# The choice of experts and the third routed tile, in another order

## The reference

```python
logits = x @ w_gate                       # 8 per token
local_gate = sigmoid(x @ w_local)
for s in range(S):
    fresh_e = argmax(logits[b, s])
    e = fresh_e if s == 0 or local_gate[b, s] < 0.5 else prev_e
    prev_e = e
    p = softmax(logits[b, s])
    out[b, s] = p[e] * (relu(x[b, s] @ w1[e]) @ w2[e])
```

## Time and profile before

| | us |
|---|---|
| median of 3 runs | 627.2 (627.11 to 627.49) |
| the profiled execution | 627.01 |
| its span, first to last instruction | 625.0 |
| PE busy | 608.4 (97%) |
| DVE busy | 410.3 (66%) |
| ACT busy | 321.1 (51%) |
| POOL busy | 176.5 (28%) |

### The profile page before, as it was taken

One profiled execution on the slowest core, in us unless ns is written; L12 is line 12 of the kernel. 1 busy time (PEld: TensorE's weight loads), 2 busy tenths in 40 slices (PEclk: granted clock), 3 DMA queues, 4 the chain that ended last, 5 costly groups with the idle time before them and its releaser, 6 DMA issues.

```text
span 625.0 us, 14720 instructions
## 1 busy us (share of the span) xinstructions
PE 608.4 (97%) x4493; PEld 506.4 (81%) x4494; DVE 410.3 (66%) x1164; ACT 321.1 (51%) x697; POOL 176.5 (28%) x241
## 2 busy tenths in 40 slices
PE   7999999999999999999999999999999999999994
PEld 6888888888788888889979878788788888888883
DVE  3777679754878797786979869948626336372621
ACT  4776779677416614632544853647516226261610
POOL 3555455600000000000000331575724412552240
PEclk9999999999999999999999999999999999999998
DMA  9987885002210010000004752887825513572000
GB/s 325 364 265 252 282 271 201 18 2 85 83 53 0 1 50 18 0 34 35 0 35 153 250 221 60 286 299 256 335 75 170 179 32 135 212 249 90 12 29 3
DMA packets 32935, 84.66 MB, mean 135 GB/s; under 512 B 4602, under 2 KB 7418, under 8 KB 32896
## 3 DMA queue, kind: packets, MB, share of 16 engines
q1 hardware_dynamic: 26816, 70.03, 32.1%
q0 software_dynamic: 3200, 8.92, 4.2%
q10 hardware_dynamic: 2880, 5.24, 2.6%
HBM read 76.04 MB, written 9.70 MB: 137 GB/s over the span
## 4 chain that ended last, share of the span: by engine, by line
PE 86%; DVE 8%; ACT 2%; issue 2%; POOL 1%; DVEq 0%; POOLq 0%; ACTq 0%
PE banks L878 22%; PE banks L880 22%; PE banks L879 22%; PE banks L754 3%; PE banks L1068 3%; PE banks L821 2%; DVE we_lo L1520 2%; PE banks L830 2%; PE banks L784 2%; PE banks L768 1%; PE banks L987 1%; PE banks L798 1%; PE banks L794 1%; PE banks L860 1%; PE banks L845 1%
## 5 line engine op out<-in xcount | busy, mean ns | idle before, releaser
L1487 DVE CUSTOM_DVE_ANT_0 product<-x,xT 128x512 f32<-128x512 f32 x120 | 77.8, 687 | 0.5 <-DMA xT<-in_w 0.4
L1784 ACT ACTIVATE prob<-neg,negmax 128x160 f32<-128x160 f32 (+1 forms) x136 | 59.1, 436 | 29.6 <-DVE negmax L1198 20.0
L1762 DVE TENSOR_SCALAR hid<-banks 128x512 f32<-128x512 f32 x34 | 23.5, 691 | 72.7 <-PE banks L880 71.6
L1891 ACT ACTIVATE k_sum<-banks 128x512 f32<-128x512 f32 (+2 forms) x40 | 21.4, 534 | 91.0 <-PE banks L880 86.3
L878 PE MATMUL banks<-we_hi,hid_hi 128*128 (+1 forms) x160 | 66.6, 416 | 0.2 <-DVE hid_lo L1595 0.2
L878 PE MATMUL banks<-we_hi,xg_hi 128*128 (+1 forms) x160 | 64.6, 404 | 1.3 <-DVE we_lo L1520 1.3
L685 POOL MEMSET xg<- 128x1024 f32 x1 | 1.0, 954 | 220.9 <-ACT k_raw L1884 220.9
L880 PE MATMUL banks<-we_hi,hid_lo 128*128 (+1 forms) x160 | 62.7, 392 | 0.0
L880 PE MATMUL banks<-we_hi,xg_lo 128*128 (+1 forms) x160 | 62.6, 391 | 0.0
L879 PE MATMUL banks<-we_lo,hid_hi 128*128 (+1 forms) x160 | 62.5, 391 | 0.0
L879 PE MATMUL banks<-we_lo,xg_hi 128*128 (+1 forms) x160 | 62.4, 390 | 0.0
(11 more groups left out here) (294 smaller groups left out, 1488.1 us busy)
## 6 DMA issues: line engine op xcount, KB each, us to landing
xT<-in_w_e SPq DMA_DIRECT2D x36, 512.0 KB, 5.0
raw_end<-in_w_e SPq DMA_DIRECT2D x36, 512.0 KB, 5.1
qk<-in_qk_t SPq DMA_DIRECT2D x32, 448.0 KB, 6.4
vw<-in_v_t SPq DMA_DIRECT2D x32, 256.0 KB, 5.2
w_raw<-in_w_mix ACTq DMA_DIRECT2D x20, 256.0 KB, 4.6
x_rows<-x SPq DMA_DIRECT2D x17, 256.0 KB, 2.0
xT<-in_w SPq DMA_DIRECT2D x8, 256.0 KB, 3.3
vz<-in_v_z SPq DMA_DIRECT2D x8, 128.0 KB, 3.6
```

The source lines that it names most:

```text
L1487: dve.tensor_tensor_reduce(product[:, k % 2, :], x2[:, t, :], w9(e), 1.0, 0.0, ALU.mult, ALU.add, dot[:, t % 2, e:e + 1]).then_inc(dotted, 1)
L1762: dve.tensor_scalar(hid[:, D * h:D * (h + 1)], ps_h[:, h, :], 0.0, None, ALU.max).then_inc(hid_ready, 1)
L1784: act.activation(prob[:, t % 2, c], neg[:, c], ACT.Exp, scale=-1.0, bias=negmax[:, t % 2, k:k + 1], accum_out=rsum[:, t % 2, k:k + 1]).the ...
L1891: act.activation(k_sum[:, f % 2, 0:w], ps_k[:, f % 2, 0:w], ACT.Relu).then_inc(k_copied, 1)
```

## The change

- First mix group, DVE: the first tile's x2 is made after the next group's k inputs and the first two steps of its r inputs, and no longer after all of them.
- Low parts of the first expert: DVE makes 2 to 5 in one run, then copies the first logits, makes the last x2, and makes parts 6 and 7 too, which POOL made before.
- PE's order around the last logits: logits, turned keeps, runs and carries each move forward by one or more steps. DVE makes the runs ahead of `rest_of_hidden(0, 0)`, and `rest_of_hidden(0, 1)` and `rest_of_rows(1)` come after the picks.
- `find_slots` comes before the last sum of `hidden(1, 1)`; DVE makes the slot numbers ahead of the next expert's low part 0, which waits for the third `rows_in` copy (it was the fourth for parts 1 to 3, and none for part 0).
- The third tile's rows are turned before the last sum of the second tile's outputs. The nine idle transposes (`keep_clock`) behind it are gone. `hidden(2, ...)` starts with three low parts and waits for the fourth before its last sum.
- ACT rounds the third tile's rows ahead of `copy_y(1)`, rounds the second expert's part 2 later, and weighs y of tiles 0 and 1 only after the rounding of the third tile's second half.
- The gates' and tables' small steps are interleaved on DVE behind `rest_of_rows(2)`; the gates are summed on PE inside the third tile's outputs (`sum_gates`), and `slot_gate` is made just before the following expert's low parts.

The core of the diff:

```diff
@@ POOL
-            pool.wait_ge(we_lo_ready, VPARTS + VPARTS)
-            last_parts(0, slice(0, 1))
@@ PE
             turn_x2(1)
-            hidden(0, first, 0, range(2, DC)).then_inc(hid_summed, 1)
-            hidden(0, first, 1, range(0, 1))
+            hidden(0, first, 0, range(2, 3))
             logits(1)
-            hidden(0, first, 1, range(1, 2))
+            hidden(0, first, 0, range(3, DC)).then_inc(hid_summed, 1)
+            hidden(0, first, 1, range(0, 2))
+            turn_keeps(final)
             pe.wait_ge(r_ready, NT + 2)
             turn_hidden(0, 0)
-            hidden(0, first, 1, range(2, 3))
-            turn_keeps(final)
-            hidden(0, first, 1, range(3, DC)).then_inc(hid_summed, 1)
+            hidden(0, first, 1, range(2, DC)).then_inc(hid_summed, 1)
+            turn_last_runs(final)
             turn_rows(1, 1, 0)
...
-            hidden(1, first, 1, range(DC // 2, DC)).then_inc(hid_summed, 1)
+            hidden(1, first, 1, range(DC // 2, DC - 1))
             find_slots()
+            hidden(1, first, 1, range(DC - 1, DC)).then_inc(hid_summed, 1)
             pe.wait_ge(y_copied, 1)
             outputs(1, 0, first, range(0, 1))
             turn_hidden(1, 1)
-            outputs(1, 0, first, range(1, FC)).then_inc(y_summed, 1)
-            turn_rows(2, 0, 1)
-            keep_clock(IDLE_TURNS // 4)
+            outputs(1, 0, first, range(1, FC - 1))
+            turn_rows(2, 0, 1)
+            outputs(1, 0, first, range(FC - 1, FC)).then_inc(y_summed, 1)
             other = slice(1, 2)
-            pe.wait_ge(we_lo_ready, VPARTS + PARTS // 2 + VPARTS)
+            pe.wait_ge(we_lo_ready, VPARTS + VPARTS + 3)
...
-            hidden(2, other, 0, range(DC)).then_inc(hid_summed, 1)
-            sum_gates()
+            hidden(2, other, 0, range(DC - 1))
+            pe.wait_ge(we_lo_ready, VPARTS + VPARTS + DC)
+            hidden(2, other, 0, range(DC - 1, DC)).then_inc(hid_summed, 1)
...
-            outputs(2, 1, other, range(1, FC)).then_inc(y_summed, 1)
+            outputs(2, 1, other, range(1, 2))
+            sum_gates()
+            outputs(2, 1, other, range(2, FC)).then_inc(y_summed, 1)
@@ DVE, first mix group
+                elif first_group(g):
+                    mix_inputs(g + 1, 0, tiles_after)
+                    mix_inputs(g + 1, 1, tiles_after, range(0, 2))
...
+                    if first_group(g) and t == 0:
+                        mix_inputs(g + 1, 1, tiles_after, range(2, DC + 1))
@@ DVE, routed tiles
             last_x2(0)
-            for j in range(2, PARTS // 2):
+            for j in range(2, VPARTS):
                 rest_of_part(0, slice(0, 1), j)
             keep_logits(0)
-            for j in range(PARTS // 2, VPARTS):
+            last_x2(1)
+            for j in range(VPARTS, PARTS):
                 rest_of_part(0, slice(0, 1), j)
-            last_x2(1)
...
             rest_of_hidden(1, 0)
+            dve.wait_ge(route_pe, 12)
+            slots(slot_of, LATER, slot_token[:, EARLY:MT])
+            dve.wait_ge(rows_in_ready, EARLY + 1)
...
             rest_of_part(1, slice(1, 2), 0)
-            dve.wait_ge(route_pe, 12)
-            slots(slot_of, LATER, slot_token[:, EARLY:MT])
-            rest_of_hidden(1, 1)
...
+            rest_of_hidden(1, 1)
-            dve.wait_ge(rows_in_ready, 2 * EARLY)
             for j in range(1, PARTS // 2):
                 rest_of_part(1, slice(1, 2), j)
             rest_of_rows(2)
...
@@ ACT
+            round_rows(2)
             copy_y(1)
-            round_rows(2)
...
-            act.wait_ge(gates_ready, 1)
-            weigh_y(0)
             relu_hidden(2, 1)
             round_rows(3)
             round_hidden(2, 1)
+            act.wait_ge(gates_ready, 1)
+            weigh_y(0)
             weigh_y(1)
             rounded_weights(2, slice(0, 1), range(3, 6))
```

More of the change, by code:

```diff
@@ L68 @@
 WARM_UP = 30
-IDLE_TURNS = 36
 HEAD_STEPS = QUADS * (4 * HEADS + 1)
@@ L1101, in _ @@
             outputs(0, 0, first, range(0, 1))
-            turn_last_runs(final)
+            turn_carries(final)
             turn_hidden(0, 1)
-            turn_carries(final)
-            outputs(0, 0, first, range(1, 3))
+            outputs(0, 0, first, range(1, 2))
             turn_chosen(final)
-            outputs(0, 0, first, range(3, 4))
+            outputs(0, 0, first, range(2, 3))
             count_picks(final)
-            outputs(0, 0, first, range(4, FC)).then_inc(y_summed, 1)
+            outputs(0, 0, first, range(3, FC)).then_inc(y_summed, 1)
             pe.wait_ge(xg_lo_ready, 3)
@@ L1701, in _ @@
             rest_of_rows(2)
+            end = ntile[0:1, 1, :].unsqueeze(1).broadcast_to([1, LATER, E])
+            after(sums)
+            sums = done(dve.tensor_scalar(gate[:, 0, :], gate[:, 0, :], EPS, None, ALU.add))
+            over = done(dve.tensor_tensor(ended[:], end, iota_tile[0:1, 0:LATER].unsqueeze(2).broadcast_to([1, LATER, E]),
+                                          ALU.is_le))
+            after(picked)
+            picked = done(dve.tensor_reduce(gate[:, 2, :], work[:], AX.X, ALU.add))
@@ new lines, in _ @@
+            none_before = done(dve.memset(tile_e[:, 0, 0:1], -1.0))
+            after(sums)
+            inverse = done(dve.reciprocal(gate[:, 1, :], gate[:, 0, :]))
+            after(over)
+            counted = done(dve.tensor_reduce(tile_e[:, 0, 1:LATER + 1], ended[:], AX.X, ALU.add))
+            after(inverse, picked)
+            gates = done(dve.tensor_tensor(gate[:, 0, :], gate[:, 2, :], gate[:, 1, :], ALU.mult))
+            after(counted)
+            this, before_it, differs, not_last = (tile_e[:, 0, 1:LATER + 1], tile_e[:, 0, 0:LATER], tile_e[:, 1, 0:LATER],
+                                                  tile_e[:, 2, 0:LATER])
@@ new lines, in _ @@
+            counted = done(dve.tensor_scalar(this, this, float(E - 1), None, ALU.min))
+            after(gates)
+            gates = done(dve.tensor_copy(gate_part[:, 0, :], gate[:, 0, :]))
+            after(none_before, counted)
+            done(dve.tensor_tensor(differs, this, before_it, ALU.subtract))
+            done(dve.tensor_scalar(table[:, EARLY:MT], this, 1.0, None, ALU.add))
+            differing = done(dve.tensor_scalar(not_last, this, float(E - 1), None, ALU.is_lt))
+            after(gates)
@@ new lines, in _ @@
+            gates = done(dve.tensor_tensor(gate[:, 1, :], gate[:, 0, :], gate_part[:, 0, :], ALU.subtract))
+            after(differing)
+            differing = done(dve.tensor_tensor(differs, differs, not_last, ALU.mult))
+            after(gates)
+            gates = done(dve.tensor_copy(gate_part[:, 1, :], gate[:, 1, :]))
+            after(differing)
+            differing = done(dve.scalar_tensor_tensor(differs, this, 2.0, differs, ALU.add, ALU.mult))
+            done(dve.tensor_scalar(table[:, 2 * MT:2 * MT + 1], ntile[0:1, 1, E - 1:E], float(EARLY), None, ALU.add))
@@ L1704, in _ @@
+            after(gates)
+            gates = done(dve.tensor_tensor(gate[:, 2, :], gate[:, 1, :], gate_part[:, 1, :], ALU.subtract))
+            after(differing)
+            dve.tensor_copy(table[:, MT + EARLY:2 * MT], differs).then_inc(tables_ready, 1)
+            after(gates)
+            gates_split = done(dve.tensor_copy(gate_part[:, 2, :], gate[:, 2, :]))
+            for j in range(PARTS // 2, VPARTS):
+                rest_of_part(1, slice(1, 2), j)
             after(gates_split)
@@ L1707, in _ @@
                                   ALU.mult)
-            for k in range(3):
+            dve.tensor_tensor(by_gate[:, :, 0, :], by_tile[:, :, 0, :], by_token(gate_part[:, 0, :], LATER), ALU.mult)
+            rest_of_hidden(2, 0)
+            for k in range(1, 3):
                 ins = dve.tensor_tensor(by_gate[:, :, k, :], by_tile[:, :, 0, :], by_token(gate_part[:, k, :], LATER), ALU.mult)
             ins.then_inc(gate_onehots_ready, 1)
-            for j in range(PARTS // 2, VPARTS):
-                rest_of_part(1, slice(1, 2), j)
+            rest_of_part(1, slice(1, 2), VPARTS)
+            rest_of_hidden(2, 1)
+            rest_of_rows(3)
             dve.wait_ge(gates_summed, 1)
+            rest_of_part(1, slice(1, 2), VPARTS + 1)
             dve.tensor_reduce(slot_gate[:, 0:EARLY], ps_chain_odd[:, 0:3 * EARLY].rearrange("p (k m) -> p m k", k=3), AX.X, ALU.add)
@@ L1716, in _ @@
                               ALU.add).then_inc(gates_ready, 1)
[L1717 to L1742, removed]
             for j in range(VPARTS):
@@ L1971, in _ @@
             round_hidden(1, 1)
+            round_rows(2)
             copy_y(1)
-            round_rows(2)
             act.wait_ge(y_summed, 3)
-            rounded_weights(2, slice(0, 1), range(0, 2))
+            rounded_weights(2, slice(0, 1), range(0, 1))
             relu_hidden(2, 0)
+            rounded_weights(2, slice(0, 1), range(1, 2))
+            round_hidden(2, 0)
             rounded_weights(2, slice(0, 1), range(2, 3))
```

(1 more changed line is left out.)

12 lines of the change are left out of this document (4 added, 8 removed).

## The result

The changed kernel takes **630.64 us** (median of 9 runs, 629.41 to 632.91) beside 627.2 for the kernel before (9 runs, 627.03 to 628.95): a ratio of 1.0053, 95% interval 1.0039 to 1.0068. It is slower, by 3.4 us, where 624.5 was forecast. The profiled execution took 630.64, its span is 628.6, 3.6 longer than before. The mean granted clock of PE is 0.990 to 0.994 in the nine runs; the profiled execution before had 0.997, and other executions of the kernel before had 0.992 to 0.997 (they are among the runs of the experiments).

A forecast was written before the change was run, and what follows sets the result against it. The prediction took the kernel to last as long as PE's own instruction stream plus its holes: 627.01 - 1.43 - 1.3 = 624.3, with the median 0.2 above, 624.5 us; range 623.4 to 629.3.

The forecast's parts named there:

- First mix group's x2: First mix group, third token tile's sum: earlier x2 on DVE removes PE's wait, gaining 1.43 us, at worst 1.2.
- Last x2 and choice: Around the last logits: x2 turned 0.50 earlier, choice 1.7 earlier, `hidden(1)` 0.5 to 1.3 us earlier; 1.3 taken.
- Slots and third tile's rows: Between second and third routed tiles: gathered rows ready in time, fillers free to drop, `hidden(2)` 2.6 us earlier.
- Gates and tables: DVE during the third tile: gates' steps add 1.1, next expert's weights reached at 401.3; fourth tile's turn 1.6 us earlier.
- the mark of a wrong forecast: Stated sign: the forecast is also wrong if DVE reaches the next expert's weights after 402.5.
- ACT and POOL behind the gates: Before the fourth tile's outputs: scatter passes, lands about 406.9, ACT loses 0.3; `outputs(3)` at 411.3, 1.3 us gained.
- the 1.3 of the sum: Gain at `outputs(3)` subtracted in the total beside the 1.43 of the first mix group; the loop behind stays as before.
- Rival 1: DVE's run of low parts locks POOL out, scatter ends at 409.0: 628.6, up to 630; chance 0.25.
- Rival 2: Scatter passes but lands 1.5 later, or gates' steps cost 2.0, delaying the fourth tile: 625.6 to 626.5; chance 0.17.

The follow-up runs named there:

- experiment 4: The kernel before without its nine filler transposes: 628.63 us, ratio 1.0021.
- experiment 2: The changed kernel with a third y buffer, so that ACT's finish of the third tile has no scatter to wait for: 625.01 us, ratio 0.9965.
- experiment 6: The changed kernel with SyncE holding the loads of the expert after the prepared one until the first scatter has landed: 624.45 us, ratio 0.9957.
- experiment 9: The changed kernel with a third y buffer, the same program repeated later on another chip: 625.39 us, ratio 0.9973.
- experiment 10: The changed kernel with both the third y buffer and the loads held until the first scatter has landed: 624.61 us, ratio 0.9961.
- experiment 1: The changed kernel with the nine filler transposes put back behind the second tile's last sum: 630.04 us, ratio 1.0044.

## Why the prediction was wrong

**First mix group's x2: right.** DVE does x2 at 162.26 in the place forecast, PE has no wait there (the matmuls follow at the 0.23 pitch through 166.69), and the part alone measured 1.4 by its ratio, against 1.43.

**Last x2 and choice: right in kind, too high.** x2 is turned at 361.40 without a wait. At `hidden(1)` the account stands at -1.75, of which 0.98 was there at the start of the stage: 0.8 gained, inside the 0.5 to 1.3 given, where I took 1.3.

**Slots and third tile's rows: two terms failed.** The first is "rows land some 2.4 after the issue. Now they land by 387.4 to 387.8". The gather's issue ended at 383.32 + 1.29 = 384.6 and PE's turn began at 388.40, 3.8 later, after 0.87 of waiting. The 2.4 came from a gather with less traffic beside it: the DMA share from 386 to 388 was 0.57 before and is 1.07 now. That this is why the rows came later is argued from the share; no run holds back the loads beside the gather. On the clock of before the third tile started 1.1 earlier (2.05 less 0.98), not 2.6. The second is the sentence "the nine fillers cost nothing to drop: the clock was full before and PE idle there anyway". That the clock had been full was the fillers' doing: without them in the old order the clock fell (experiment 4), and in the profiled execution of the new order it fell too and cost 1.65. It isn't the main loss, though. Experiments 2, 6, 9 and 10 have no fillers and end at 624.45 to 625.39, and experiment 1 has them and ends at 630.0.

**Gates and tables: 0.8 to 1.2 too early, and then the clock.** DVE came to the next expert's weights at 403.06 (404.0 on the clock of before), past the 402.5 that I had named as the mark of a wrong forecast. Its timeline has 1.82 of idle before 397.55, waiting for sums at the lower clock; in experiments 1, 2 and 6, with the clock full, ACT's weighing starts at 400.93, 400.78 and 400.79, where the routed stage starts 1.46, 1.69 and 1.34 sooner than in the kernel before. On the clock of before that is 402.1 to 402.5, 0.8 to 1.2 later than the 401.3 of the forecast; in the changed kernel it is 403.18 + 0.98 = 404.2, and the further 1.7 to 2.0 goes with TensorE's clock, which cost 1.65 there.

**ACT and POOL behind the gates: the step that failed.** "If it gets through at the next instruction it ends at 404.4, lands at about 406.9": it did get through, in 1.48, and landed 6.0 after the issue's end, not 2.5. This 2.5 was taken from a gather in a quieter stretch, though in the same prediction DVE's low parts run from 401.3 on and each of them releases a load of 512 KB. The forecast asked which engine might hold the scatter up, and not which transfers lay beside it; only the two rivals added 1.5 for a slow landing. The list was complete otherwise: the queue behind the wait (y(2), parts 6 and 7, the rounding) is what held PE for 3.4.

**The whole miss, in the profiled execution.** The forecast put `outputs(3)` at 411.3 - 1.43 = 409.87, and it came at 416.51, 6.6 later: 3.5 for the landing, 1.65 for the clock at 390, 0.6 in attention, where the kernels are the same, and some 0.9 for the rows and the gates that came later than forecast. The last part is there without the others too: where the scatter is out of the way the new order brings 0.4 to 0.8, not the 1.3 of the sum.

**The rivals.** Rival 1 named 628.6 to 630 and so nearly the right size, but for the wrong reason: POOL was not locked out, and its own mark (a scatter that ends after 407.5) was not met, for it ended at 406.3 (407.3 on the clock of before). Rival 2 had the right place, a slow landing, at 1.5 instead of 3.5. The range's upper end, 629.3, was 1.3 short, since no case put the slow landing and the clock together.

**What stays open.** How the 1.65 at 390 and the hole at 416 share the loss isn't settled for executions other than the profiled one, and none of the other profiles of the new order has the fall at 390: experiment 1 shows that when the first is filled the clock can fall behind the second. Why the clock fell after 0.87 and 0.76 of idle, and not after 0.71 and 0.76 in experiment 2 or 0.37 and 0.76 in experiments 6 and 10, no run here tells.

## What to carry to other kernels

Give a transfer's landing the price of the traffic beside it: list what the load queue issues in the same few microseconds, above all for small scatters that free a buffer. When a step is moved later, look at what it now travels with, not only at which engine it waits for; here 2 to 4 us of delay put a 256 KB scatter among 2 MB of weights, and one extra buffer, or holding the loads until it had landed, turned a loss of 3.4 into a gain of 1.7 to 2.7, of which 1.4 is the mix part's. And a filler that keeps the clock is costed by taking it out, not by seeing that the clock is full.

## What the runs showed of the hardware that was not expected

An indirect scatter of 128 rows of 2 KB landed 7.45 us after its issue began beside 512 KB loads (7.63 in experiment 1), and within 3.4 without them (experiment 6). An issue on POOL asked in the second of six back-to-back DVE subtractions of two inputs took 1.48; in the kernel before, one asked in the first of six had taken 7.13. PE's clock fell to half in one execution of the changed kernel after two holes of less than 0.9 us each, 1.4 us apart.
